# Issuing a prefetch ahead of the output stores on one DMA-issuing engine, in a fused FFT convolution and two-MoE kernel

## The reference

```
X = rfft(x, axis=1); y = irfft(X * (filt_r + 1j*filt_i), n=3008, axis=1)   # x: 4 x 3008 x 256
z = relu(y @ w_in)**2 @ w_out                                             # 12032 tokens, 256 -> 2048 -> 256
g = z @ w_gate; v = z @ w_val                                             # 256 -> 1536
out = (g * sigmoid(g) * v) @ w_out2                                       # 1536 -> 256
```

## Time and profile before

| | |
|---|---|
| time, median of 3 runs | 2443.48 us (2442.09 to 2445.52) |
| profiled execution: its own time | 2448.92 us |
| profiled execution: span from first to last instruction | 2447.1 us |
| mean granted TensorE clock | 0.98 of full |
| PE busy | 2355.1 us (96%) |
| DVE busy | 1601.0 us (65%) |
| ACT busy | 1274.4 us (52%) |

### The profile page before, as it was taken

How to read it: one execution, slowest core, us unless ns; L and a number is a source line. 1 busy time by engine, 2 the same in 40 slices (tenths; PEclk the granted TensorE clock), 3 DMA queues, 4 the chain that set the end, 5 groups by cost and what they waited for, 6 DMA issues and landing times.

```text
span 2447.1 us, 31292 instructions
## 1 busy us (share of the span) xinstructions
PE 2355.1 (96%) x10581; PEld 1919.8 (78%) x10581; DVE 1601.0 (65%) x2707; ACT 1274.4 (52%) x2468; POOL 61.2 (3%) x124
## 2 busy tenths in 40 slices
PE   8899999999999999999999989898898988989999
PEld 4688888888888888888888778787787877877787
DVE  2567766676667766566558667676676766766776
ACT  4566655566556655555444445454454544545454
POOL 0100000000000000000000000000000000000000
PEclk9899999999999999999999999999999999999999
DMA  9643333333332332110111010100101001010000
GB/s 257 202 127 109 116 100 106 89 112 105 107 114 82 111 109 68 33 34 27 31 32 65 22 35 1 35 9 27 35 1 35 9 26 35 1 35 23 13 18 18
DMA packets 95423, 153.74 MB, mean 63 GB/s; under 512 B 10080, under 2 KB 48416, under 8 KB 94976
## 3 DMA queue, kind: packets, MB, share of 16 engines
q1 hardware_dynamic: 82112, 132.96, 17.4%
q0 software_dynamic: 13152, 18.78, 3.2%
HBM read 101.89 MB, written 49.81 MB: 62 GB/s over the span
## 4 chain that ended last, share of the span: by engine, by line
PE 93%; DMA 4%; SPq 1%; issue 1%; DVE 1%; ACT 1%; ACTq 0%; DVEq 0%
PE psum L1450 31%; PE psum L1452 30%; PE psum L1451 30%; DMA zq_raw<-z_scratch 2%; PE psum L1552 1%; DMA filt0b<-filt 1%; PE psum L1554 1%; PE psum L1461 1%; SPq L695 1%; DMA B_scratch<-b_out 0%; DVE d_full L1310 0%; SPq L562 0%; SPq L557 0%; PE psum L1504 0%; DMA w<-w_full 0%
## 5 line engine op out<-in xcount | busy, mean ns | idle before, releaser
L1217 DVE SCALAR_TENSOR_TENSOR prod<-psum,act_out 128x512 f32<-128x512 f32 (+1 forms) x384 | 261.0, 680 | 400.3 <-ACT act_out L917 399.8
L917 ACT ACTIVATE act_out<-psum 128x512 f32<-128x512 f32 (+1 forms) x384 | 226.1, 589 | 463.4 <-PE psum L1452 462.8
L1450 PE MATMUL psum<-g_hi,m_hi 128*128 128x512 f32 (+1 forms) x768 | 306.0, 398 | 1.9 <-ACT z_raw L820 1.8
L1450 PE MATMUL psum<-v_hi,m_hi 128*128 128x512 f32 (+1 forms) x768 | 298.7, 389 | 1.5 <-DVE v_lo L1115 1.5
L1452 PE MATMUL psum<-v_hi,m_lo 128*128 128x512 f32 (+1 forms) x768 | 297.6, 387 | 0.0
L1451 PE MATMUL psum<-v_lo,m_hi 128*128 128x512 f32 (+1 forms) x768 | 297.6, 387 | 0.0
L1452 PE MATMUL psum<-g_hi,m_lo 128*128 128x512 f32 (+1 forms) x768 | 296.9, 387 | 0.0
L1451 PE MATMUL psum<-g_lo,m_hi 128*128 128x512 f32 (+1 forms) x768 | 296.7, 386 | 0.0
L1115 DVE TENSOR_TENSOR g_lo<-prod,g_hi 128x512 fp32r<-128x512 f32 (+1 forms) x408 | 270.6, 663 | 1.1 <-ACT g_hi L820 1.0
L820 ACT ACTIVATE g_hi<-prod 128x512 fp32r<-128x512 f32 (+1 forms) x408 | 248.5, 609 | 0.9 <-DVE prod L1251 0.9
L820 ACT ACTIVATE g_hi<-g_full 128x512 fp32r<-128x512 f32 x264 | 165.9, 629 | 126.8 <-DVE g_full L1331 126.6
(11 more groups left out here) (125 smaller groups left out, 4262.0 us busy)
## 6 DMA issues: line engine op xcount, KB each, us to landing
filt_in<-filt SPq DMA_DIRECT2D x36, 512.0 KB, 3.8
z_scratch<-z_raw SPq DMA_DIRECT2D x23, 512.0 KB, 2.9
b_in<-B_scratch SPq DMA_DIRECT2D x122, 96.0 KB, 2.8
zq_raw<-z_scratch SPq DMA_DIRECT2D x44, 256.0 KB, 4.1
B_scratch<-b_out SPq DMA_DIRECT2D x38, 256.0 KB, 2.1
A_scratch<-a_out SPq DMA_DIRECT2D x50, 192.0 KB, 2.1
x_in<-x SPq DMA_DIRECT2D x48, 192.0 KB, 2.9
a_in<-A_scratch SPq DMA_DIRECT2D x36, 256.0 KB, 3.4
```

What stands on the lines that cost most here:

```text
L917: nc.scalar.activation(act_out[n % 2][:, 0:w], psum[:, n % 3, 0:w], ACT.Relu).then_inc(relu_done, 1)
L1217: nc.vector.scalar_tensor_tensor(out=prod[n % 2][:, 0:w], in0=psum[:, n % 3, 0:w], scalar=0.0, in1=act_out[n % 2][:, 0:w], op0=ALU.max, op ...
L1450: nc.tensor.matmul(dst, wh, vh, start=start, stop=False, skip_group_check=True)
```

## The change

In SP's loop over the double tiles, `load_zq(k + 1)` is called before the two `store_quad` of double k-1, and no longer after them. No instruction is added or removed, and no wait: each call keeps its own.

```
             for k in range(DOUBLES):
+                if k + 1 < DOUBLES:
+                    load_zq(k + 1)
                 if k:
                     store_quad(k - 1, 1)
                     store_quad(k - 1, 0)
-                if k + 1 < DOUBLES:
-                    load_zq(k + 1)
             store_quad(DOUBLES - 1, 1)
             store_quad(DOUBLES - 1, 0)
```

## The result

The changed kernel takes **2359.4 us** (median of 4 runs, 2358.64 to 2360.24), against 2442.78 us (2439.55 to 2445.52) of the kernel before in 4 runs. The ratio is 0.9659, with a 95% interval of 0.9642 to 0.9676: 83.4 us less. The forecast was 2359.7 us.

What follows compares the result with a forecast made beforehand. PE, busy 96%, was taken as the bound, losing time to late fetches in nine doubles: 62.6 us idle plus 21.2 us clock, 83.8 us. From 2443.5 this gave 2359.7 us, range 2354 to 2367, stated to 2368.

Steps and rivals of the forecast that it cites:

- When the fetch starts: On SP at double 9: fetch issued at about 2247.2 after p4(107), some 13.8 us earlier than 2261.03.
- When it lands: At double 9: landing about 2253.8, or 2255.4 at longest, before `sum_t` at 2258.8; margin 5.0 or 3.4 us.
- What is late next: After `sum_t` in double 9: `right_val(109)` still waits for p7 at 2259.65, so PE meets no wait.
- The fetch beside full work: The 1 MB fetch now moves beside busy PE: cost between nothing and 2 us in all, taken as nothing.
- The rival of a fetch that slows its neighbours: Fetch in step 12k slows matmuls, `right_val` and ACT's copies, 10.5 us a double: 2454 us; chance 0.02.
- The sum: Nine stalled doubles, 908.49 us, against nine unstalled, 824.67: loss 83.8 us, 62.6 PE idle and 21.2 left for the clock.
- The 5.4 us: Profiled execution's excess over the median, place unknown; if all in the nine stalls, gain 78 us and time 2365.

Runs made afterwards that it cites:

- Experiment 1: Changed kernel with the fetch between the two pairs of stores, behind the right tile's and ahead of the left's: 2360.92 us, ratio 0.9668.
- experiment 5: Kernel before, stores still ahead of the fetch, but VectorE makes the four differences in steps 2, 3, 4 and 4 of a double: 2356.52 us, ratio 0.9654.
- experiment 2: Kernel before plus 28 useless matmuls on TensorE ahead of the stalling p4 in doubles 1 to 9: 2422.59 us, against 2440.78 before in the same job.
- held for p6: Changed kernel, but the fetch waits for p6 of step 12k+1 instead of p4 of the step before the double: 2397.2 us, ratio 0.9813.
- held for p3: Changed kernel, but the fetch waits for p3 of step 12k+1 instead of p4 of the step before the double: 2426.06 us, ratio 0.9934.
- held for p1: Changed kernel, fetch ahead of the stores but waiting for p1 of step 12k+2: 2448.89 us, ratio 1.0029.
- experiment 3: The run held for p6: changed kernel, fetch waiting for p6 of step 12k+1: 2397.2 us, ratio 0.9813.
- experiment 8: The run held for p1: changed kernel, fetch ahead of the stores but waiting for p1 of step 12k+2: 2448.89 us, ratio 1.0029.

## Why the prediction was right

**When the fetch starts.** Forecast: 13.8 us earlier. Measured against `d_full` of the first step: 9.01 + 4.89 = 13.9.

**When it lands.** Forecast: a margin of 3.4 to 5.0 us. `sum_t` shows no wait for the fetches of doubles 2 to 10 in the changed kernel. From the first issue it starts 11.5 to 11.6 us later, and by then the last of the four blocks had been there for 5.4 to 6.5 us. The fetches between 1440 and 2300 us, each from its own issue to its landing:

```profile
DMA to landing us min/median/max: 2.6/3.4/4.3
```

The margin was larger than forecast, because I had carried over the 6.6 us from the first issue to `sum_t` of the kernel before; now it took 5.0 to 6.2. Experiment 1 agrees: it issued the fetch 6.7 us later than the change does, and VectorE then waited 1.3 us. The 1.2 us that TensorE has in hand beyond it were not in my working.

**What is late next.** Nothing, as forecast: `d_full` of step 109 waits 0.29 us for p7, and the step is 7.67 us long where I had said at most 7.65. These 0.02 us are not the fetch's: in experiment 5, where it is issued only 9.0 us after `d_full` of step 12k, this step is 7.67 us long in the odd doubles and 7.65 in the even ones, just as here. My limit was too tight.

**The fetch beside full work.** I took nothing, between bounds of 0 and 2 us. Nine doubles took 824.74 us, and nine times the undisturbed one is 824.67. The rival of a fetch that slows its neighbours is refuted in this trace. The rule of the Trainium skill that a DMA and an engine cannot contend for SBUF (SBUF — State Buffer, the section on the two separate sides) agrees with it.

**The sum.** 83.8 us were forecast and 83.75 found in the doubles. Its split into 62.6 us of idleness and 21.2 of clock was only the remainder of a subtraction until experiment 2, which gave 19.65 us for the clock. The subtraction gave the clock 1.5 us too much: the record of a matmul is 0.40 us long, but at the full clock the next one starts 0.231 us after it, so each of the nine gaps reads 0.17 us short of what was lost. With them the idleness is 64.1 us and the clock 19.65. (That both ways agree to the second decimal is chance: VectorE's waits in the nine doubles were 1.1 us shorter in experiment 2, 75.9 against 77.0.) Half of the 5.12 us at half clock, by the rule of the Trainium skill (TensorE: Matmul & The Clock Gate, its list of terms), would be 23 us in nine stalls, an estimate; the measurement lies below both, and nearer to the rows' 21.2.

That the time itself came within 0.3 us is partly luck: the four runs span 1.6 us, and the median of the kernel before was 2443.48 us in my rows and 2442.78 beside the result.

**The 5.4 us** by which the profiled execution of before stood above its median were not in the stalls, as far as the traces show: the start-up stretch varies by as much. Step 0 came at 1351.17 us in that trace, at 1346.31 in that of the changed kernel, and between 1343.0 and 1348.5 in the other eight.

What my expectations of the experiments got wrong were two sizes: the landing, 5.9 to 6.1 us in the mean when stores follow the fetch instead of 5.0, and the price of the clock after short stalls.

## What to carry to other kernels

On an engine that works in order, ask of each transfer what its own condition is and when that is met, and what stands before it that is met later; here 13.8 us lay between the two in each of nine doubles and cost 9.3, with the DMA engines nearly idle (a share of 0.07 over the nine doubles). The cure can be at either end: to issue the fetch earlier, or to put its first consumer a step later in the engine's order, which served as well. When the stall is on TensorE, cost it as idle time plus what the clock takes afterwards, here nearly another third (19.65 us to 64.1).

## What the runs showed of the hardware that I had not expected

In the mean of nine stalls, the price of the clock does not grow with the idle time from 4.5 to 7.5 us. In each kernel the loss of a double less its idle time leaves this for the clock (loss: the nine doubles less 824.74 us, divided by nine; idle: PE's waits, divided by nine; the last column includes the 0.17 us by which a gap reads short):

| kernel | idle us | loss us | left for the clock us |
|---|---|---|---|
| held for p6 | 2.53 | 4.47 | 1.94 |
| held for p3 | 4.52 | 7.36 | 2.84 |
| before | 6.96 | 9.31 | 2.35 |
| held for p1 | 7.46 | 9.89 | 2.43 |

So a short stall is relatively the dearest: 2.5 us of idleness cost 4.5. The means hide that single stalls of nearly the same idle time differ: in the kernel before, double 3 idled 7.1 us and took 10.2 us more than the undisturbed 91.64, double 8 idled 6.9 and took 8.6 more, so 3.1 and 1.7 us are left for the clock. What decides between them no run here shows.

At still shorter stalls the clock can hold. The first double (k = 0) idled 1.8 us in the trace of before and in that of the hold for p3, and the clock fell. In the changed kernel it idled 1.6 us, in experiments 1, 2, 3 and 8 between 1.5 and 1.7, and when the changed kernel was run again 1.9 us, and it did not fall. From `d_full` of step 0 to that of step 2 it took 17.4 us in the two where it fell, and 15.6 to 15.9 in the others.
